# The last row tile read from PSUM, a branch hint on VectorE and bounds on a loaded count

## The reference

```python
x = np.ascontiguousarray(attn_out.transpose(0, 2, 1, 3)).reshape(B * S, H * D)
h = x @ w_in                                     # 512 -> 2048
g = np.where(pos, h, np.where(neg, 0.0, (h + beta) ** 2 / (4.0 * beta)))
x = g @ w_out                                    # 2048 -> 512

skip_score = x @ w_skip
do_compute = skip_score > 0
out = x.copy()
xc = x[do_compute]
e_idx = np.argmax(xc @ w_gate, axis=1)           # one of 8 experts
...                                              # y: gated expert output
out[do_compute] = xc + y
```

## Time and profile before

| what | value |
|---|---|
| median of 3 executions | 506.68 us (506.3 to 506.68) |
| profiled execution, its own time | 506.3 us |
| its span | 504.5 us |
| mean granted TensorE clock | 0.999 |
| PE busy | 493.8 us, 98% |
| DVE, ACT, POOL busy | 253.7, 194.3, 212.7 us |
| DMA | 42.13 MB, mean 84 GB/s |

### The profile page before, as it was taken

One profiled execution on the slowest core, in us unless ns is written; L12 is line 12 of the kernel. 1 busy time (PEld: TensorE's weight loads), 2 busy tenths in 40 slices (PEclk: granted clock), 3 DMA queues, 4 the chain that ended last, 5 costly groups with the idle time before them and its releaser, 6 DMA issues.

```text
span 504.5 us, 8886 instructions
## 1 busy us (share of the span) xinstructions
PE 493.8 (98%) x3427; PEld 426.3 (85%) x3427; DVE 253.7 (50%) x595; ACT 194.3 (39%) x435; POOL 212.7 (42%) x235
## 2 busy tenths in 40 slices
PE   8899999999999999999999999999999999999996
PEld 4588888889988888888888888888998898888895
DVE  5976656733335636676524666652445342332322
ACT  4974655543223324343433343433322222222222
POOL 0679876662223224465433555652222312222221
PEclk9999999999999999999999999999999999999999
DMA  8993210103001204102110521000300017850001
GB/s 274 335 388 128 73 45 38 52 2 125 1 1 48 74 23 174 57 25 71 59 48 1 173 81 34 1 2 17 123 3 1 1 40 295 290 170 1 2 1 64
DMA packets 18975, 42.13 MB, mean 84 GB/s; under 512 B 2054, under 2 KB 3920, under 8 KB 18932
## 3 DMA queue, kind: packets, MB, share of 16 engines
q1 hardware_dynamic: 18580, 41.13, 24.0%
q10 hardware_dynamic: 256, 0.41, 0.2%
q0 software_dynamic: 96, 0.02, 0.0%
HBM read 32.94 MB, written 8.78 MB: 83 GB/s over the span
## 4 chain that ended last, share of the span: by engine, by line
PE 89%; DVE 4%; ACT 3%; DMA 1%; issue 1%; POOL 0%; SPq 0%; DVEq 0%; ACTq 0%
PE bank L1046 39%; PE bank L1030 39%; PE bank L832 4%; PE bank L869 3%; PE bank L849 2%; ACT prob_first L1559 1%; DMA qk<-in_qk_dram 1%; PE bank L973 1%; PE bank L954 1%; DVE sum_terms L1191 1%; DVE prob_first L1165 1%; DVE prob L1181 1%; ACT g_hi L1689 0%; DVE bank L1174 0%; DVE row_max L1169 0%
## 5 line engine op out<-in xcount | busy, mean ns | idle before, releaser
L1792 POOL TENSOR_TENSOR g_lo<-act_f,g_hi 128x384 fp32r<-128x384 f32 x96 | 97.5, 1016 | 196.7 <-ACT g_hi L1689 196.3
L1680 ACT ACTIVATE act_f<-act_f,half_col 128x384 f32<-128x384 f32 x96 | 59.1, 616 | 200.7 <-DVE act_f L1416 200.7
L1416 DVE TENSOR_SCALAR act_f<-bank 128x384 f32<-128x384 f32 x96 | 53.4, 556 | 146.4 <-PE bank L1030 141.5
L1030 PE MATMUL bank<-x_hi,win_hi 128*128 128x384 f32 x384 | 87.7, 347 | 0.6 <-DVE act_f L1419 0.6
L1046 PE MATMUL bank<-wout_hi,g_hi 128*128 128x512 f32 x285 | 85.0, 406 | 0.0
L1689 ACT CAST g_hi<-act_f 128x384 fp32r<-128x384 f32 x96 | 49.2, 513 | 92.1 <-DVE act_f L1419 91.8
L1030 PE MATMUL bank<-x_hi,win_lo 128*128 128x384 f32 x384 | 83.9, 337 | 0.0
L1030 PE MATMUL bank<-x_lo,win_hi 128*128 128x384 f32 x384 | 83.1, 334 | 0.0
L1046 PE MATMUL bank<-wout_lo,g_hi 128*128 128x512 f32 x285 | 81.1, 393 | 0.0
L1046 PE MATMUL bank<-wout_hi,g_lo 128*128 128x512 f32 x285 | 81.0, 392 | 0.0
L1030 PEld LDWEIGHTS bank<-x_hi,win_hi 128*128 128x128 f32 x384 | 66.7, 188 | 8.3 <-issue 1.5
(11 more groups left out here) (131 smaller groups left out, 420.7 us busy)
## 6 DMA issues: line engine op xcount, KB each, us to landing
w_early<-in_w_dram SPq DMA_DIRECT2D x4, 2048.0 KB, 9.0
qk<-in_qk_dram SPq DMA_DIRECT2D x12, 592.0 KB, 4.9
out_dram<-y_rows SPq DMA_DIRECT2D x18, 256.0 KB, 2.6
win_raw<-in_w_in_dram SPq DMA_DIRECT2D x16, 256.0 KB, 8.8
wout_raw<-in_w_out_dram SPq DMA_DIRECT2D x16, 256.0 KB, 8.9
y_dram<-y_rows SPq DMA_DIRECT2D x15, 256.0 KB, 3.0
v<-in_v_dram SPq DMA_DIRECT2D x6, 384.0 KB
v<-in_v_dram SPq DMA_DIRECT2D x6, 288.0 KB
```

What stands on the lines that cost most here:

```text
L1030: mm = pe.matmul(h_ps[s % 2][:, 0:CH], w[:, f, P * k:P * (k + 1)], x[:, k, cols], start=(at == 0), stop=(at == len(order) - 1))
L1416: dve.tensor_scalar(tile, h_ps[s % 2][:, 0:CH], -1.0, 1.0, ALU.max, ALU.min).then_inc(clip_ready, 1)
L1680: act.activation(tile, tile, ACT.Square, bias=half_col[:, 0:1], scale=0.5).then_inc(square_ready, 1)
L1792: pool.tensor_tensor(g_lo[:, s % RING, :], act_f[:, s % 2, :], g_hi[:, s % RING, :].bitcast(F32), ALU.subtract).then_inc(g_lo_ready, 1)
```

## The change

It has four parts. (1) The load of the count states that the value lies in 0 to `N`; the register load is then followed by two more sequencer instructions, on all five engines. (2) For the last tile DVE takes its score from PSUM as soon as `l2_done` is there, as for the tiles before; ACT copies that tile after DVE's score. (3) In `keep_sums` DVE waits for `row_skips` as ACT does already, in four chunks, before each of its two copies. (4) DVE gets a branch hint at step 88, as PE has one.

```diff
@@ for_tiles
-            n_left = eng.value_load(left_i[0:1, 0:1])
+            n_left = eng.value_load(left_i[0:1, 0:1], min_val=0, max_val=N)
@@ last_skips
                     if t < CT - 1:
                         dve.wait_ge(rows_done, t + 1)
-                        rows = y_ps[t]
                     else:
-                        wait_rows(dve, CHUNKS - 1, t)
-                        rows = y_rows[:, t, :]
+                        dve.wait_ge(l2_done, STEPS)
                     q = CT * (CHUNKS - 1) + t
-                    dve.tensor_tensor_reduce(out=skip_terms[:, :], in0=rows[:, :], in1=w_skip_sb[:, :], scale=1.0,
+                    dve.tensor_tensor_reduce(out=skip_terms[:, :], in0=y_ps[t][:, :], in1=w_skip_sb[:, :], scale=1.0,
@@ keep_sums on DVE
                     if c > 0:
                         dve.wait_ge(y_stored[t], 32 * c)
+                        dve.wait_ge(row_skips, CT * c)
@@ the loop over the steps on DVE
             for s in range(STEPS):
+                if s == HINT_STEP:
+                    the_end_is_likely = dve.mark_branch_hint_location()
@@ end of DVE
-            for_tiles(dve, first, tile)
+            for_tiles(dve, first, tile, the_end_is_likely)
@@ keep_last_sums on ACT
-                    if t < CT - 1:
-                        act.wait_ge(row_skips, CT * c + t + 1)
-                    else:
-                        act.wait_ge(l2_done, STEPS)
+                    act.wait_ge(row_skips, CT * c + t + 1)
```

## The result

| | before | after |
|---|---|---|
| time, median (lowest to highest), 6 runs each | 506.57 (505.93 to 506.68) | 509.12 (508.52 to 510.26) |
| ratio to before, with its 95% interval | 1 | 1.0054 [1.0042, 1.0065] |
| profiled execution, time and span | 506.3, 504.5 | 509.0, 507.1 |
| start of PE's last matmul of `last_outputs` | 499.46 | 499.97 |
| from there to the end of the span (the **tail**) | 5.0 | 7.1 |

The change made the kernel slower by 0.5%, outside the predicted range of 505.8 to 507.2. It is the case that the prediction called rival B. For the ratios further down: of 94 executions of the kernel before that were timed beside the experiments, 8 took 507.4 to 508.2, and they move a ratio where they hardly move a median, so the two are read together.

A forecast was written before the change was run, and what follows sets the result against it. PE, busy 98%, bounds the kernel; only a 5 us tail changes. The count comes 1.22 earlier, checks take 0.3, and the store's 0.3 later end takes most of the rest: 506.68 - 0.2 = 506.5 us, range 505.8 to 507.2.

The forecast's parts named there:

- rival B: At the closing branch, a queue whose target is not held waits 2.1 for a fetch; on DVE 507.9 us, chance 0.04.
- the sum: Adding up the tail: DVE and POOL drained at 503.3, SP last; gain 0 to 0.3 us, taken as 0.2.
- the rule: At the closing branch, the Trainium skill: a target outside the two pages held needs a DMA fetch; counted as no cost.
- ACT's 0.31: In the tail, ACT's third copy waits for DVE's readout and starts 0.31 us later, at 500.90 for 500.59.
- SP's passage at 503.6: SP's first closing wait, passed at 503.6 before; landing delay or branch restart left open, up to 0.2 delay counted.
- A: At the end, the last store lands later than 2.2: 507.0 us at 2.6, 507.8 at 3.4; chance 0.12.
- C: At the end, the landing does not hold SP up and the gain goes through: 0.9 gained, 505.8 us; chance 0.03.
- D: In the tail, checks cost more than 0.35 or the hint disturbs, so nothing is gained: 506.7 us; chance 0.07.
- the marks named as wrong: Profile signs against the forecast: DVE or POOL draining after SP, late or long score, branch stall over 1 us, moved last matmul.

The follow-up runs named there:

- e14: The changed kernel with DVE's branch hint moved from step 88 to right before the last scores; 508.89 us, ratio 1.0045.
- e5: The kernel before with only the last tile's score read from PSUM and ACT's copy behind it; 506.21 us, ratio 0.9986.
- e6: The kernel before with only the bounds on the loaded count; 506.91 us, ratio 1.0.
- e8: The kernel before with the score from PSUM and the `keep_sums` waits, without bounds and hint; 506.07 us, ratio 0.9984.
- e10: The changed kernel without the bounds on the loaded count; waits, score from PSUM and hint stay; 505.88 us, ratio 0.9989.
- e13: The changed kernel with DVE's branch hint at step 60 in place of 88, list length unchanged; 506.14 us, ratio 0.9988.
- +12: The kernel before with twelve increments of an unused semaphore in DVE's list at step 88, nothing else; 507.48 us, ratio 1.0014.
- +9: The kernel before with nine increments of an unused semaphore in DVE's list at step 88, nothing else; 509.79 us, ratio 1.006.
- e4: The changed kernel, hint included, with sixteen increments of an unused semaphore in DVE's list at step 88; 506.67 us, ratio 1.0017.

## Why the prediction was wrong

**The failed step** is the time that the sum gives DVE from branch to drain. Part 1 has "drain 0.6 later", taken over from the earlier trace rows; it was 3.56. The clause in part 4 that lets it stand is that no branch of five stalls in the trace of before, "so the sum is the same with the rule and without it, as long as this stays so". The rows show five branches at their places of then, and say nothing of a place seven instructions on. The place could have been estimated: by the DMA view and DVE's own instructions in the trace of before, the branch comes 115 instructions behind the q14 packet at 404.1. Its target is some 120 to 130 further on by the kernel's list (no trace shows this, as these instructions are jumped). That makes 235 to 245, where two fetches of 124 to 131 hold about 256, a cover of some 10 to 20 with an error of several, against 7 added; measured, it was 5. Such a count would not have forecast the stall, but it would have shown that the border is near and that 0.04 was too low. I had the +7 and the rule, and did not count.

**Rival B** had the mechanism word for word, at a chance of 0.04. Its price was a DMA's way, 2.1; a fetch takes 3.0 more than the branch without one (3.54 to 3.67, less 0.6; 3.3 more in e14). B's own sum gave 507.9. By the same working with 3.0 on the drain it is 508.8, and the median was 509.12.

**Part 2** was right in its working, all but one reading: score, count, ACT's 0.31 (copy of tile 2 at 501.35 - 499.97 = 1.38 behind the last matmul's start, forecast 1.44), the store, SP last. Its gain was too small by half (0.44, not 0.2), as SP's passage at 503.6 was the branch's restart and not the landing.

**Part 1** was sized well on DVE (0.33, forecast 0.3). Not foreseen: the loads of the count take 0.66 on DVE and 0.75 to 0.78 on ACT, POOL and PE in after, where they took 0.54 and 0.47 to 0.50. They do so in e5 as well, without bounds, and not in e6: it comes with the earlier load, not with the check. From load to branch ACT takes 1.04 in after, before 0.50. All of this hides behind the landing.

**Part 3** was zero as forecast (e8), and PE's cover at a chunk's end is unchanged.

**Rivals A, C, D.** The last store landed in 2.0 to 2.1, so A did not come. C did not either, as SP waits for the landing. D's checks are hidden by it.

Of the marks named as wrong, "a branch with over 1 us behind it" is the one that appeared.

## What to carry to other kernels

An edit that adds only a few instructions to one queue moves every later branch of this queue in its fetch blocks; ahead of a taken branch to a far target, count where it stands between the instruction fetches of the trace (the packets of the kind "instruction", against the queue's own count), and price a miss at 3 us. When a change loses a few microseconds that none of its parts explains, pad the old kernel by the same number of instructions: if it loses the same, the cause is the place. Here the versions that leave out two of the new instructions, or give the hint a block earlier, are 0.1% faster than before in place of 0.5% slower (e10 and e13: 505.88 and 506.14 us, their intervals just under 1). The count has an error of several instructions; here it would have warned and not decided.

## What the runs showed of the hardware

- A taken branch whose target is not at hand stands DVE for 3.54 to 3.91 us; one with its target at hand for 0.58 to 0.63. The fetch that the branch asks for leaves its packet 1.04 to 1.06 behind the branch. Where the fetch was already under way at the branch, the gap was 1.59 (+12).
- The fetch ahead is tied to the progress of the queue, not to free time: at +9 no packet of DVE's stands between 405.2 and its branch at 504.6, though DVE sat idle for over 1 us 23 times in between.
- A branch hint at 331 us, ahead of DVE's last regular fetch at 398, removed the stall; at 457.7 and 495.0, behind that fetch, it did not, with 45 and 7.7 us of lead. Three places are tried, in one kernel.
- On DVE, ACT, POOL and PE the load of a value from SBUF into a register takes 0.65 to 0.78 us where it starts 0.1 to 0.2 behind the issue of the last store, and 0.47 to 0.55 where it starts 1.6 to 1.7 behind it. Which of these neighbours does it was not separated.
- Open: the 0.7 to 1.0 us that a fetch asked for by the branch takes longer from packet to restart than the one at +12, the four slower runs of ten of e4, the exact point between +9 and +12, and whether the other queues have such borders near (only DVE's list was padded).
